# Attention and expert adapters on one core: how many whole-row stores may be on their way, row 5 and the end of row 7 stored in pieces, and a new order of the engines' work

## The chip, the cores and the metric

The kernel runs on one core of one Trainium2 chip. The metric is device time in microseconds (us) of one execution; less is better. The core's engines are PE (TensorE, matrix products; its weight loads are listed as PEld), ACT (ScalarE), DVE (VectorE), POOL (GpSimd) and SP (SyncE), and 16 DMA engines carry its transfers. Here POOL issues the loads of q, k and v, and SP issues the stores of the output.

## The reference, cut to what matters

```python
def _attn_ref(q, k, v):                      # (8, 8, 576, 64): batch, head, position, channel
    scores = np.matmul(q, k.transpose(0, 1, 3, 2)) / np.sqrt(D)
    # heads 0-3: rel = i - j in [0, 32); heads 4-7: rel in [0, 128) and rel % 4 == 0
    scores = np.where(mask, scores, -1e9)
    attn = softmax(scores)
    return np.matmul(attn, v)

def _moe_ref(x, w_gate, A, B):               # x: (8 * 576, 512), 8 experts of rank 16
    logits = x @ w_gate
    # the two largest logits of each token, softmax over these two -> w
    # out = x + sum over the two experts e of w_e * (x @ A[e]) @ B[e]
```

## The kernel before, in words

A *row* r (0 to 7) is one batch element: 576 tokens by 512 channels of float32, 1152 KB of output. A row has two halves g, the plain heads (g = 0) and the dilated heads (g = 1). All work is cut into named operations with an engine, a body and a list of operations that they wait for (`Program.add`, line 88). For a row r and half g:

- `L..`, `Lw..`, `Lq..`, `Lv..` load q, k and v from float32 in HBM to bfloat16 on the chip, issued by POOL. There are four input buffers, so row r uses that of row r - 4. Row 7 comes in eight pieces (lines 293 to 298): `Lq7gh` for queries and keys, `Lv7gh` for values. All of the pieces but `Lv700` and `Lv701` are put into the list `late`, and every store waits for that list.
- `S0`, `S1` (PE, scores), `E0`, `E1` (ACT, exponentials), `V` (PE, times the values), `R` and `N` (DVE, reciprocal and normalisation into the output tile X[r]), `B` (POOL, a bfloat16 copy of X[r]; the last part of row 7 is `Bx7` on ACT).
- `T`, `U` (PE, transposes), `C`, `Cd`, `Cp` (ACT, copies of them), `Z0`, `Z1` (PE, x times A and the gate), `Y0`, `Y1` (ACT, copies), then the gate's statistics on DVE: `m0`, `m1`, `s12`, `top`, `tt`, with `th` on ACT, `g2` on DVE; `gz` (POOL, gated z), `G` (PE, transposes), `gc` and `gn` (ACT, copies).
- `D0`, `D1`, `D2` (PE, times B): the first 1024 columns of half 0, those of half 1, and the last 128 columns of both halves. `A0`, `A1`, `A2` add them to X[r], on DVE; of rows 4 to 7 `A2` is done on POOL after a copy `dx` on ACT (lines 576 to 579). In the rows 5, 6 and 7 (`SHARED`, line 35) `A0` takes the first 512 columns only, and `A3` on POOL the next 512, after a copy `dy` on ACT (lines 554 to 559). In row 7 `D70` is for `A70` and `D73` for `A73`.
- `O` stores X[r], issued by SP, in the order O1 O0 O2 O3 O4 O5 O61 O60 O71 O70. Rows 0 to 5 go out whole (line 592) when `A0`, `A1`, `A2` (and `A3`) of the row are done. The rows 6 and 7 go out in halves of 576 KB (line 596); a half g waits for `Ag`, `A2` and, for g = 0, for `A3`.

The text PLAN (lines 602 to 633) gives the order of all operations. Each engine runs its own in that order, so an operation whose inputs are late holds up all behind it on its engine. The number after @ is the operation's first PSUM bank of eight; an operation that takes a bank waits for the users of the one that had it before (`ordered`, lines 96 to 114). Line 110 adds a wait to each store of a whole row:

```python
            if name[0] == "O":
                if len(name) == 2:
                    o.deps = o.deps + stores[-2:-1]
                stores.append(name)
```

So a whole-row store waits until the last store but one ahead of it has landed: O2 waits for O1, O3 for O0, O4 for O2, O5 for O3. SP issues in order, so a store that waits holds up those behind it.

Of the kernel before, what the change touches and what calls it, by code (L numbers as in the profile page):

```python
# [13 lines left out]
B, H, S, D = 8, 8, 576, 64  # L14
# [14 lines left out]
XG = 1152  # L29
# [52 lines left out]
class Program:  # L82
# [5 lines left out]
    def add(self, name, eng, work, emit, deps=(), bank=None):  # L88
        assert name not in self.ops, name
        o = Op(name, eng, work, emit, [d for d in deps if d is not None], bank)  # L90
        self.ops[name] = o
        if bank is not None:
            bank.users.append(name)
        return name

    def ordered(self, text):


        out, held, stores = [], [[] for _ in range(8)], []
        for word in text.split():  # L100
            name, _, at = word.partition("@")
            o = self.ops[name]
            if o.bank is not None and o.bank.users[0] == name:
                o.bank.at = int(at)
                for b in range(o.bank.at, o.bank.at + o.bank.size):
                    o.deps = o.deps + held[b]
                    held[b] = list(o.bank.users)
            if name[0] == "O":
                if len(name) == 2:
                    o.deps = o.deps + stores[-2:-1]  # L110
                stores.append(name)
            out.append(o)
        assert len(out) == len(self.ops) == len(set(o.name for o in out))
        return out
# [52 lines left out]
def program(nc=None, qkv=None, aw=None, bt=None, con=None, out=None):  # L167
    scale = 1.0 / float(D) ** 0.5
    pg = Program()
    add = pg.add  # L170

    def sb(name, shape, dt):
        return nc.alloc_sbuf_tensor(name, shape, dt) if nc is not None else None

    IN = [sb(f"in{i}", [128, SW], BF) for i in range(SLOTS)]
    X = [sb(f"x{r}", [128, 2 * XG], FP) for r in range(B)]
# [13 lines left out]
    G2 = [sb(f"g2{i}", [128, 5, 8], FP) for i in range(2)]  # L190
# [75 lines left out]
    qk_ready, v_ready, late = {}, {}, []  # L266
# [321 lines left out]
        adapters(r)  # L588
    for r in range(B):
        more = [f"A{r}3"] if r in SHARED else []  # L590
        if r < B - 2:
            add(f"O{r}", "SP", ("dma", 128, 9216), lambda r=r: [nc.sync.dma_start(out=out[r], in_=X[r][:, :])],
                [f"A{r}{n}" for n in range(3)] + more + late)
        else:
            for g in range(2):
                add(f"O{r}{g}", "SP", ("dma", 128, 4608), lambda r=r, g=g: [nc.sync.dma_start(
                    out=out[r][:, XG * g : XG * g + XG], in_=X[r][:, XG * g : XG * g + XG])],
                    [f"A{r}{g}", f"A{r}2"] + more * (1 - g) + late)
    return pg


PLAN = """
pz0 wz warm@4 F1@1 awf btf vz00 pz2 con vz10 Lk00 Lk01 Lv00 Lv01
S000@6 vz01 vz11 tab cc1 cd3 vz20 cc0 vz21 cd2 cd0 L11 pz1 E000
F2@1 L10 cd1 S100@4 S101@6 E100 E101 L2 Lw2 S001@2 E001 V00@4 R00 N00 V01@1
L3 Lw3 R01 F0@0 xz0 B00 N01 B01 T00@4 vz30 L4 Lw4 pz3 C00 S111@5 E111
awc S011@2 U0@0 T01@7 E011 V11@3 Cd0 Cp0 S010@1 C01 R11 vz31 E010 N11
Z00@0 Y00 m00 Z10@6 Y10 m10 S110@4 B11 s120 E110 tt0 th0 top0 V10@2
g20 gz0 T11@5 R10 N10 btc G0@1 gc0 D01@6 B10 gn0 D00@0 C11 xz1
U1@4 Cd1 Cp1 T10@5 C10 A01 A00 S121@6 E121 S120@3 S021@1 Z01@0 E021 Z11@5  # L610
Y01 m01 Y11 m11 L5 Lw5 s121 S020@1 D02@0 V21@5 E120 top1 tt1 th1 g21
E020 A02 V20@0 R21 N21 R20 gz1 G1@5 gn1 F3@6 S130@6 N20 gc1 B21 E130
S031@3 D12@2 E031 S030@0 D10@5 T21@7 E030 C21 A12 S131@3 B20 V30@0 A10 E131
U2@7 T20@6 R30 N30 Cp2 B30 L6 Lw6 V31@3 Cd2 C20 Z02@7 Y02 Z12@1 R31
N31 B31 T30@2 D11@6 Y12 C30 S041@4 A11 E041 S141@2 S140@6 m02 E141 S040@0
m12 s122 tt2 U3@5 Cp3 th2 E040 top2 Cd3 g22 gz2 V41@2 T31@0 E140
C31 V40@5 R41 N41 Z03@2 G2@0 Y03 gn2 Z13@1 gc2 R40 Y13 N40 B40
S051@2 D20@4 E051 A20 m13 S151@6 E151 Lq700 S050@0 S150@2 E150 m03 s123 V51@5
top3 tt3 T40@3 th3 Lq701 E050 C40 B41 g23 T41@4 C41 R51 Lq710 V50@0
N51 R50 D22@5 N50 U4@7 gz3 Cd4 Cp4 G3@6 gn3 D21@3 gc3 A22 A21  # L620
Z04@7 Y04 B50 Lq711 S060@0 D32@2 Z14@7 S161@5 m04 E060 Y14 m14 E161 s124
S160@0 A32 Lv710 T50@7 E160 D30@3 S061@5 top4 V60@0 A30 tt4 R60 C50 Lv711
O1 E061 B51 T51@3 N60 C51 V61@4 th4 g24 R61 N61 U5@7 S171@2 Cp5
Cd5 S070@0 Z05@7 E171 E070 Z15@6 Y05 S170@2 S071@4 Y15 Lv700 m05 m15 top5
Lv701 B60 gz4 E170 E071 s125 G4@0 B61 D31@6 tt5 th5 gn4 V70@1 T60@4
A31 gc4 V71@5 U6@0 C60 O0 g25 O2 gz5 G5@4 Cp6 Cd6 R70 N70
B70 T61@2 D41@0 D42@3 R71 N71 gn5 A41 C61 dx4 gc5 B71 Bx7 D40@5
Z06@2 Y06 Z16@4 Y16 A40 m06 A42 D52@3 m16 s126 dx5 top6 U7@7 Cp7
Cd7 tt6 T71@1 Cx7 C71 T70@4 D51@5 A52 th6 g26 A51 D50@0 A50 C70
gz6 Z07@2 Z17 m07 m17 s127 tt7 dy5 G6@5 gc6 O3 D61@0 th7 gn6  # L630
D62@7 A53 top7 O4 dx6 g27 D60@5 gy7 gz7 A62 dy6 O5 A61 A63
O61 G7@3 H7 gm7 gn7 gc7 D72@0 dx7 A72 D71@1 A60 D73@6 O60 A71
D70@7 O71 A70 dy7 A73 O70
"""

_INS = ["qkv", "aw", "bt", "con"]
# [64 lines left out]
```

## Time and profile before

| | us |
|---|---|
| median of 3 runs | 101.34 |
| lowest and highest | 100.81, 101.72 |
| profiled execution: span from the first to the last instruction | 99.2 |
| what lies around the span (101.34 - 99.2) | 2.1 |

| engine | busy us | share of the span |
|---|---|---|
| PE | 81.6 | 82% |
| ACT | 71.0 | 72% |
| DVE | 62.3 | 63% |
| POOL | 54.6 | 55% |

The profile tells no time of its own for the profiled execution beside its span. Its views count time from the span's start. A line of a group names the source line, the engine, the operation, output <- input and the number of instructions. In the page's slices one column is a fortieth of the span, 2.48 us; a busy digit is in tenths.

### The profile page before, as it was taken

The page shows a single profiled execution, that of the slowest core. Times are in us where ns is not written, and L with a number is a line of the kernel's source. Part 1 is how long each engine was busy: PE and PEld are TensorE (multiplying, and loading weights), DVE is VectorE, ACT ScalarE, POOL GpSimd, SP SyncE. Part 2 cuts the span into 40 slices and gives each one's busy share as a digit, 9 for nine tenths or more (in the row PEclk, how much of TensorE's full clock was granted, in tenths as well). Part 3 has the DMA queues.
Part 4 walks back from the last instruction along what each step waited for, and adds up shares of the span by engine and source line. Part 5 has one row for each costly group of instructions (what it writes and reads, how often), then busy time and mean ns, then how long its engine had stood idle before and what let it go on. Part 6 is the DMA issues. An engine that isn't in the chain of part 4 may idle for free.

```text
span 99.2 us, 3611 instructions
## 1 busy us (share of the span) xinstructions
PE 81.6 (82%) x1587; PEld 59.9 (60%) x1587; DVE 62.3 (63%) x138; ACT 71.0 (72%) x123; POOL 54.6 (55%) x73
## 2 busy tenths in 40 slices
PE   3999969959569989999897979999799989766200
PEld 2443457548356765779676859878687878545100
DVE  5770007706468189359746697779676999979700
ACT  5195494399938983896997679989689899757200
POOL 5999900880549136404942297099085574637800
PEclk9999999999999999999999999999999999999975
DMA  2999999999999999999999999999979988979991
GB/s 33 300 204 208 207 214 226 201 217 220 211 211 211 214 219 213 219 216 206 210 217 212 224 212 214 210 204 175 198 264 412 415 353 360 426 297 401 420 422 76
DMA packets 5807, 24.50 MB, mean 247 GB/s; under 512 B 800, under 2 KB 928, under 8 KB 5024
## 3 DMA queue, kind: packets, MB, share of 16 engines
q0 software_dynamic: 3920, 14.23, 71.9%
q1 hardware_dynamic: 1728, 9.77, 23.9%
q10 hardware_dynamic: 144, 0.28, 1.0%
q8 instruction: 12, 0.20, 0.7%
q14 instruction: 3, 0.02, 0.1%
HBM read 29.07 MB, written 9.44 MB: 388 GB/s over the span
## 4 chain that ended last, share of the span: by engine, by line
PE 57%; ACT 18%; DVE 9%; DMA 5%; issue 3%; POOL 2%; POOLq 0%
PE ps L213 49%; ACT p L351 11%; PE ps L414 5%; DMA out_dram<-x 5%; DVE x L551 4%; DVE x L390 3%; ACT xt L424 2%; PE ps L504 1%; ACT zs L472 1%; POOL x L559 1%; ACT in L263 1%; POOL xb L397 1%; PE ps L438 1%; ACT xt L427 1%; DVE top L492 1%
## 5 line engine op out<-in xcount | busy, mean ns | idle before, releaser
L397 POOL CAST xb<-x 128x1152 bf16<-128x1152 f32 (+1 forms) x16 | 18.3, 1144 | 25.4 <-DVE x L390 25.4
L351 ACT ACTIVATE p<-ps 128x960 bf16<-128x960 f32 (+1 forms) x32 | 27.6, 899 | 4.2 <-PE ps L213 4.1
L213 PE MATMUL ps<-in,p 128*64 128x130 bf16 (+1 forms) x416 | 21.5, 221 | 3.7 <-ACT p L351 3.1
L390 DVE TENSOR_TENSOR x<-ps,rec 128x1152 f32<-128x1152 f32 x16 | 21.7, 1358 | 0.5
L213 PEld LDWEIGHTS ps<-in,p 128*64 128x64 bf16 (+1 forms) x416 | 17.1, 104 | 7.2 <-ACT p L351 4.1
L551 DVE TENSOR_TENSOR x<-x,ps 128x1024 f32<-128x1024 f32 (+1 forms) x16 | 17.5, 1116 | 3.4 <-PE ps L213 3.4
L387 DVE RECIPROCAL rec<-ps 128x18 f32<-128x18 f32 x16 | 4.3, 270 | 17.5 <-PE ps L213 17.3
L213 PE MATMUL ps<-warm 128*128 128x512 f32 x22 | 13.1, 737 | 1.5 <-DVE warm L217 1.5
L499 POOL TENSOR_TENSOR gz<-zs,g 128x640 bf16<-128x640 f32 x7 | 8.9, 1275 | 9.4 <-DVE g L494 9.4
L213 PEld LDWEIGHTS ps<-in 64*64 64x64 bf16 x576 | 10.9, 106 | 2.9 <-issue 0.9
L213 PE MATMUL ps<-in 64*64 64x96 bf16 (+1 forms) x576 | 11.9, 201 | 0.7 <-issue 0.7
L273 POOL DMA_DIRECT2D in<-in_qkv_dram x22 | 11.8, 581 | 0.8 <-POOLq L684 0.8
L213 PE MATMUL ps<-aw,xt 128*128 128x136 bf16 x160 | 11.2, 223 | 0.1
L424 ACT COPY xt<-ps 128x1024 bf16<-128x1024 bf16 x8 | 8.1, 1011 | 3.4 <-PE ps L414 3.3
L213 PEld LDWEIGHTS ps<-aw,xt 128*128 128x128 bf16 x160 | 9.6, 98 | 0.9 <-ACT xt L424 0.4
L414 PE MATMUL ps<-one,xb 128*128 128x128 bf16 x128 | 9.6, 219 | 0.6 <-issue 0.5
L414 PEld LDWEIGHTS ps<-one,xb 128*128 128x128 bf16 x128 | 7.6, 97 | 2.0 <-POOL xb L397 0.7
L213 PEld LDWEIGHTS ps<-warm 128*128 128x128 f32 x22 | 4.8, 235 | 6.6 <-issue 5.0
L427 ACT COPY xt<-ps 128x1024 bf16<-128x1024 bf16 x7 | 7.2, 1033 | 1.5 <-PE ps L414 1.5
L213 PE MATMUL ps<-bt,gn 128*128 128x256 bf16 (+1 forms) x48 | 6.8, 263 | 1.6 <-ACT gn L523 0.8
L213 PE MATMUL ps<-bt,gc 128*128 128x256 bf16 (+1 forms) x48 | 6.6, 255 | 1.5 <-ACT gc L520 1.5
L472 ACT COPY zs<-ps 128x408 f32<-128x408 f32 (+1 forms) x14 | 5.9, 457 | 2.0 <-PE ps L213 2.0
(55 smaller groups left out, 101.8 us busy)
## 6 DMA issues: line engine op xcount, KB each, us to landing
out_dram<-x SPq DMA_DIRECT2D x6, 1152.0 KB, 6.1
in<-in_qkv_dram POOLq DMA_DIRECT2D x5, 1152.0 KB, 22.1
in<-in_qkv_dram POOLq DMA_DIRECT2D x10, 292.5 KB, 23.1
in<-in_qkv_dram POOLq DMA_DIRECT2D x10, 288.0 KB, 8.2
out_dram<-x SPq DMA_DIRECT2D x4, 576.0 KB, 3.8
in<-in_qkv_dram POOLq DMA_DIRECT2D x10, 146.2 KB, 8.1
in<-in_qkv_dram POOLq DMA_DIRECT2D x2, 434.2 KB, 13.7
awf<-in_aw_dram ACTq DMA_DIRECT2D x1, 272.0 KB, 3.8
```

Of the source, the lines that this page charges most:

```text
L213: return nc.tensor.matmul(o, lhsT=lhsT, rhs=rhs, start=start, stop=stop, skip_group_check=True)
L273: nc.gpsimd.dma_start(out=IN[r % SLOTS][half(a), at : at + n], in_=qkv[r, a, :, at - 2 * VB * a : at - 2 * VB * a + n],)
L351: return [nc.scalar.activation(p[:, :, :].rearrange("p h (s c) -> p h s c", c=PER)[:, :, b0 : b0 + nb, 0:SEG], PS[:, k.at : k.at + 2, 0 : ...
L387: rc = add(f"R{tag}", "DVE", ("el", 60), lambda: [nc.vector.reciprocal(rec[:, :].rearrange("p (b i) -> p b i", b=3), PS[:, k.at : k.at + 3 ...
L390: nm = add(f"N{tag}", "DVE", ("el", XG), lambda: [nc.vector.tensor_tensor(X[r][:, XG * g : XG * g + XG].rearrange("p (b i n) -> p b i n", ...
L397: add(f"B{tag}", "POOL", ("el", cut), lambda: [nc.gpsimd.tensor_copy(XB[r % 2][:, g, 0:cut], X[r][:, XG * g : XG * g + cut])], [nm] + free)
L414: nc.tensor.transpose(tp[j][:, 128 * u : 128 * u + 128], xb[:, g, 256 * u + 128 * j : 256 * u + 128 * j + 128], ident())
L424: return [nc.scalar.copy(xt[:, 0:2, 0:S].rearrange("p j (c i) -> p j c i", c=C)[:, :, :, 0:128], tp.rearrange("p j (i c) -> p j c i", c=C))]
L427: return [nc.scalar.copy(xt[:, 2:4, 0:512], tp)]
L472: zc.append(add(f"Y{st}{r}", "ACT", ("el", len(us) * ZW), lambda us=us, k=k: [nc.scalar.copy(zs[:, us[0] : us[-1] + 1].rearrange("p u n -> ...
L499: return [en.tensor_tensor(GZ[i][:, us[0] : us[0] + n, :].rearrange("p u (e r) -> p u e r", e=E), zv()[:, us[0] : us[0] + n, 0:ER].rearran ...
L551: return [nc.vector.tensor_tensor(v, v, PS[:, k.at : k.at + nk].rearrange("p b n -> p (b n)"), ALU.add)]
```

## The change

1. A whole-row store waits for the last store but two ahead of it: O3 waits for O1 and O4 for O0; O2 waits for no store.
2. Row 5 goes out in two halves, O51 (after `A51` and `A52`) ahead of O50 (after `A50`, `A52` and `A53`). Row 7's half 0 goes out in two pieces, O70 (its first 512 columns, after `A70` alone) and O70b (640 columns, after `A72` and `A73`). The order is O1 O0 O2 O3 O4 O51 O50 O61 O60 O70 O71 O70b.
3. PLAN is drawn up anew. The order of every engine is the same up to row 5's second scores (S150); up to there only banks differ. Behind it orders and banks differ.

```diff
@@ ordered
-                    o.deps = o.deps + stores[-2:-1]
+                    o.deps = o.deps + stores[-3:-2]
@@ program, stores
-        if r < B - 2:
+        if r < B - 3:
             add(f"O{r}", "SP", ("dma", 128, 9216), lambda r=r: [nc.sync.dma_start(out=out[r], in_=X[r][:, :])],
                 [f"A{r}{n}" for n in range(3)] + more + late)
         else:
             for g in range(2):
-                add(f"O{r}{g}", "SP", ("dma", 128, 4608), lambda r=r, g=g: [nc.sync.dma_start(
-                    out=out[r][:, XG * g : XG * g + XG], in_=X[r][:, XG * g : XG * g + XG])],
-                    [f"A{r}{g}", f"A{r}2"] + more * (1 - g) + late)
+                parts = ((0, XG, [f"A{r}{g}", f"A{r}2"] + more * (1 - g)),)
+                if (r, g) == (B - 1, 0):
+                    parts = ((0, 512, [f"A{r}0"]), (512, XG, [f"A{r}2"] + more))
+                for i, (x0, x1, made) in enumerate(parts):
+                    add(f"O{r}{g}" + "b" * i, "SP", ("dma", 128, 4 * (x1 - x0)), lambda r=r, x0=XG * g + x0, x1=XG * g + x1: [
+                        nc.sync.dma_start(out=out[r][:, x0:x1], in_=X[r][:, x0:x1])], made + late)
@@ PLAN, from row 5's second scores on
-S051@2 D20@4 E051 A20 m13 S151@6 E151 Lq700 S050@0 S150@2 E150 m03 s123 V51@5
-top3 tt3 T40@3 th3 Lq701 E050 C40 B41 g23 T41@4 C41 R51 Lq710 V50@0
-N51 R50 D22@5 N50 U4@7 gz3 Cd4 Cp4 G3@6 gn3 D21@3 gc3 A22 A21
-Z04@7 Y04 B50 Lq711 S060@0 D32@2 Z14@7 S161@5 m04 E060 Y14 m14 E161 s124
-S160@0 A32 Lv710 T50@7 E160 D30@3 S061@5 top4 V60@0 A30 tt4 R60 C50 Lv711
-O1 E061 B51 T51@3 N60 C51 V61@4 th4 g24 R61 N61 U5@7 S171@2 Cp5
-Cd5 S070@0 Z05@7 E171 E070 Z15@6 Y05 S170@2 S071@4 Y15 Lv700 m05 m15 top5
-Lv701 B60 gz4 E170 E071 s125 G4@0 B61 D31@6 tt5 th5 gn4 V70@1 T60@4
-A31 gc4 V71@5 U6@0 C60 O0 g25 O2 gz5 G5@4 Cp6 Cd6 R70 N70
-B70 T61@2 D41@0 D42@3 R71 N71 gn5 A41 C61 dx4 gc5 B71 Bx7 D40@5
-Z06@2 Y06 Z16@4 Y16 A40 m06 A42 D52@3 m16 s126 dx5 top6 U7@7 Cp7
-Cd7 tt6 T71@1 Cx7 C71 T70@4 D51@5 A52 th6 g26 A51 D50@0 A50 C70
-gz6 Z07@2 Z17 m07 m17 s127 tt7 dy5 G6@5 gc6 O3 D61@0 th7 gn6
-D62@7 A53 top7 O4 dx6 g27 D60@5 gy7 gz7 A62 dy6 O5 A61 A63
-O61 G7@3 H7 gm7 gn7 gc7 D72@0 dx7 A72 D71@1 A60 D73@6 O60 A71
-D70@7 O71 A70 dy7 A73 O70
+G2@4 Y03 gn2 Z13@2 gc2 R40 Y13 N40 B40 S051@0 D20@4 E051 A20 m13 S151@2
+E151 Lq700 S050@6 S150@0 B41 T41@2 E050 m03 s123 tt3 E150 th3 Lq710
+Lq711 top3 g23 V51@3 C41 U4@7 T40@6 gz3 R51 Cp4 V50@0 N51 Lq701 Cd4 B51
+Lv710 R50 N50 C40 G3@7 Lv711 Lv701 gn3 Z14@4 Y14 D21@5 A21 B50 O1 Lv700
+gc3 S060@3 E060 Z04@7 D22@0 A22 O0 O2 Y04 m04 m14 top4 S161@4 s124 tt4
+E161 S160@1 E160 th4 g24 gz4 S061@6 T51@3 D30@4 A30 E061 C51 V60@0 R60
+U5@6 Cp5 N60 Cd5 T50@7 C50 D32@3 V61@4 A32 R61 N61 S171@2 E171 S070@0
+E070 Z05@7 Y05 Z15@2 Y15 m05 m15 top5 s125 B60 tt5 S170@0 E170 D31@6
+S071@4 B61 A31 O3 th5 g25 V70@1 E071 G4@0 gn4 gz5 R70 N70 gc4 T60@4 C60
+V71@5 U6@2 Cp6 R71 Cd6 T61@1 C61 B70 N71 D42@0 G5@2 gc5 D41@3 A41 dx4
+A42 gn5 Z06@6 Y06 m06 Z16@7 Y16 T70@3 B71 m16 s126 Bx7 C70 top6 tt6 th6
+D40@0 A40 g26 gz6 T71@4 U7@2 Cd7 C71 Cx7 D51@6 A51 D50@0 Cp7 A50 O4
+D52@5 dx5 Z07@2 dy5 Z17 G6@5 gc6 D61@0 A52 O51 m07 m17 s127 tt7 th7 top7
+g27 gz7 gy7 gn6 D62@7 A61 D60@5 G7@3 A53 O50 H7 dx6 A62 O61 dy6 A63 gn7
+D70@0 gm7 gc7 D72@7 dx7 A60 O60 A70 O70 D71@4 A71 A72 O71 D73@3 dy7 A73
+O70b
```

## Rows read from the trace of the kernel before

**Rows 1.** The page: DMA busy in tenths and its rate in 40 slices; the instruction queue's transfers.

```profile
DMA  2999999999999999999999999999979988979991
GB/s 33 300 204 208 207 214 226 201 217 220 211 211 211 214 219 213 219 216 206 210 217 212 224 212 214 210 204 175 198 264 412 415 353 360 426 297 401 420 422 76
q8 instruction: 12, 0.20, 0.7%
```

**Rows 2.** Windows: length; PE, PEld, DVE, ACT, POOL busy us (count); clock, DMA share, GB/s.

```profile
73.00:86.00 13.00, 12.17 (x235) 9.84 (x227) 11.42 (x28) 12.45 (x26) 7.93 (x9) 1.00 0.95 394
76.00:81.00 5.00, 4.83 (x87) 3.92 (x84) 4.67 (x8) 4.63 (x10) 2.42 (x2) 1.00 1.04 433
81.40:82.40 1.00, 1.00 (x18) 0.96 (x17) 1.00 (x2) 1.00 (x3) 0.98 (x2) 1.00 0.40 166
87.80:88.90 1.10, 0.57 (x4) 0.31 (x4) 0.81 (x5) 1.10 (x3) 0.03 (x1) 1.00 0.44 184
97.00:97.50 0.50, 0.00 (x0) 0.00 (x0) 0.00 (x0) 0.00 (x0) 0.00 (x0) 0.50 0.42 166
97.50:98.00 0.50, 0.00 (x0) 0.00 (x0) 0.00 (x0) 0.00 (x0) 0.00 (x0) 0.50 0.07 28
```

**Rows 3.** One source line in windows, stores: all whole rows, O2, O4, O5, O70.

```profile
L592 SPq DMA_DIRECT2D out_dram<-x x6: 332/332/976, 72.4 to 87.9; - x6
DMA to landing us min/median/max: 4.4/6.1/8.6
...
L592 SPq DMA_DIRECT2D out_dram<-x x1: 332/332/332, 76.9 to 76.9; - x1
DMA to landing us min/median/max: 7.0/7.0/7.0
...
L592 SPq DMA_DIRECT2D out_dram<-x x1: 332/332/332, 83.9 to 83.9; - x1
DMA to landing us min/median/max: 6.3/6.3/6.3
...
L592 SPq DMA_DIRECT2D out_dram<-x x1: 333/333/333, 87.9 to 87.9; - x1
DMA to landing us min/median/max: 5.0/5.0/5.0
...
L596 SPq DMA_DIRECT2D out_dram<-x x1: 332/332/332, 94.3 to 94.3; - x1
DMA to landing us min/median/max: 4.1/4.1/4.1
```

**Rows 4.** What SP waited for from 77.3 to 84 us, and from 84.3 to 88 us: total, times, longest.

```profile
SPq L140 <- DMA out_dram<-x: 6.2, 2, 4.2
...
SPq L140 <- POOL x L559: 3.6, 1, 3.6
```

**Rows 5.** Timeline of DVE, then ACT, then POOL's A53, then SP's issue of O61.

```profile
76.37 1.22 DVE L551 TENSOR_TENSOR x<-x,ps 128x1024 f32<-128x1024 f32 x1 [0.20 <-PE ps L213]
...
80.94 2.34 DVE L551 TENSOR_TENSOR x<-x,ps 128x1024 f32<-128x1024 f32 x2
83.23 0.30 DVE L484 MAX8 mx<-zs 128x8 f32<-128x8 f32 x3
...
84.55 0.19 DVE L489 SCALAR_TENSOR_TENSOR tt<-zs,s 128x40 f32<-128x40 f32 x1
...
82.64 0.84 ACT L472 COPY zs<-ps 128x408 f32<-128x408 f32 x2
...
86.56 1.27 POOL L559 TENSOR_TENSOR x<-x,in 128x512 f32<-128x512 f32 x1
...
90.73 0.33 SPq L596 DMA_DIRECT2D out_dram<-x  x1
```

**Rows 6.** Timeline of POOL: B50, then three of row 7's loads.

```profile
64.49 1.14 POOL L397 CAST xb<-x 128x1152 bf16<-128x1152 f32 x1 [2.54 <-DVE x L390]
65.58 1.63 POOL L273 DMA_DIRECT2D in<-in_qkv_dram  x3
```

More of the change, by code:

```diff
@@ L599, in program @@
     return pg
 PLAN = """
[L603 to L616, printed above, removed]
@@ L617 @@
-C31 V40@5 R41 N41 Z03@2 G2@0 Y03 gn2 Z13@1 gc2 R40 Y13 N40 B40
-S051@2 D20@4 E051 A20 m13 S151@6 E151 Lq700 S050@0 S150@2 E150 m03 s123 V51@5
-top3 tt3 T40@3 th3 Lq701 E050 C40 B41 g23 T41@4 C41 R51 Lq710 V50@0
-N51 R50 D22@5 N50 U4@7 gz3 Cd4 Cp4 G3@6 gn3 D21@3 gc3 A22 A21
-Z04@7 Y04 B50 Lq711 S060@0 D32@2 Z14@7 S161@5 m04 E060 Y14 m14 E161 s124
-S160@0 A32 Lv710 T50@7 E160 D30@3 S061@5 top4 V60@0 A30 tt4 R60 C50 Lv711
-O1 E061 B51 T51@3 N60 C51 V61@4 th4 g24 R61 N61 U5@7 S171@2 Cp5
-Cd5 S070@0 Z05@7 E171 E070 Z15@6 Y05 S170@2 S071@4 Y15 Lv700 m05 m15 top5
@@ L633 @@
-D70@7 O71 A70 dy7 A73 O70
+pz0 wz warm@0 F1@3 awf btf vz00 pz2 con vz10 Lk00 Lk01 Lv00 Lv01 S000@4
+vz01 vz11 tab cc1 cd3 vz20 cc0 vz21 cd2 cd0 L11 pz1 E000 F2@7 L10 cd1
+S100@5 S101@0 E100 E101 L2 Lw2 S001@3 E001 V00@5 R00 N00 V01@1 L3 Lw3
+R01 F0@4 xz0 B00 N01 B01 T00@4 vz30 L4 Lw4 pz3 C00 S111@6 E111 awc
+S011@3 U0@2 T01@7 E011 V11@4 Cd0 Cp0 S010@1 C01 R11 vz31 E010 N11 Z00@3
+Y00 m00 Z10@0 Y10 m10 S110@1 B11 s120 E110 tt0 th0 top0 V10@2 g20 gz0
+T11@0 R10 N10 btc G0@5 gc0 D01@6 B10 gn0 D00@1 C11 xz1 U1@4 Cd1 Cp1
@@ new lines @@
+T10@0 C10 A01 A00 S121@6 E121 S120@3 S021@1 Z01@0 E021 Z11@7 Y01 m01 Y11
+m11 L5 Lw5 s121 S020@1 D02@0 V21@5 E120 top1 tt1 th1 g21 E020 A02 V20@0
+R21 N21 R20 gz1 G1@4 gn1 F3@5 S130@6 N20 gc1 B21 E130 S031@3 D12@2 E031
+S030@0 D10@5 T21@7 E030 C21 A12 S131@3 B20 V30@0 A10 E131 U2@7 T20@6 R30
+N30 Cp2 B30 L6 Lw6 V31@3 Cd2 C20 Z02@6 Y02 Z12@2 R31 N31 B31 T30@0 D11@6
+Y12 C30 S041@2 A11 E041 S141@4 S140@6 m02 E141 S040@0 m12 s122 tt2 U3@5
+Cp3 th2 E040 top2 Cd3 g22 gz2 V41@2 T31@0 E140 C31 V40@5 R41 N41 Z03@1
```

## The prediction

> **What bounds the kernel now.** I read the page's slices first. The 16 DMA engines are busy in nearly every slice [rows 1]: up to about 72 us with loads at some 210 GB/s, then with stores at 400 GB/s and more. The clock of PE stays at its full level until PE has nothing left to do [rows 2]. So the second view is of transfers: when each store is issued and when it lands [rows 3]. The first leaves at 72.4, when row 7's loads have landed, the last at 94.3, and it lands at 94.3 + 4.1 = 98.4; the span ends 0.8 later, at 99.2. Eight rows of 1152 KB (1.18 MB) at the undisturbed 433 GB/s of 76 to 81 us [rows 2] take 8 x 2.72 = 21.8 us. From the first issue to the last landing it was 26.0. What lies between is what a change of the stores can win.
>
> Third, the windows with little DMA [rows 2]. From 81.4 to 82.4 the share is 0.40, so 0.6 us is empty; from 87.8 to 88.9 it is 0.44, another 0.6. The view of SP's waits says why [rows 4]: O3 waited 4.2 us for O0, which lands 8.6 us after its issue, the longest of the six [rows 3]; O5 waited 3.6 us for POOL's A53, which ends at 86.56 + 1.27 = 87.8 [rows 5].
>
> Fourth, the end. In 97.0 to 97.5 the share is 0.42, in 97.5 to 98.0 it is 0.07, about one engine of 16 [rows 2]. So 15 engines have no data left at about 97.2 and one goes on. The landings tell that this one hardly waited before: O4 lands at 83.9 + 6.3 = 90.2, O5 at 87.9 + 5.0 = 92.9, O70 at 98.4: 2.7 us for one row, 5.5 for two, the pure transfer time. And O2 lands at 76.9 + 7.0 = 83.9 although most engines were empty from 81.5 on. A store lands with its slowest engine, and the slowest one is not idle in the gaps. Why it is behind can be bounded: 12 instruction transfers take 0.7% of 16 engines' 99.2 us [rows 1], so 11.1 / 12 = 0.93 us each, on one engine, while the other 15 go on.
>
> The Trainium skill ("Runtime: NRT & Kernel Launch", Instruction fetch mechanics) says that such blocks of 16 KiB come over a DMA queue of the sequencer's own, mostly hidden. The size agrees (0.20 MB in 12); hidden it would be for the engine that executes, and by it nothing would be added for a laggard, which takes 0.45 off the sum below.
>
> So two things share the bound: the DMA engines' work, and the times at which the compute engines hand over the rows 4 to 7.
>
> **A rule for the end.** O5 left at 87.9 with three rows to go. 3 x 2.72 = 8.2, and the 15 engines ended at about 97.2: the remaining 1.1 is 0.85 until the data moves (87.8 to 88.9 is empty for 0.62 after a last remnant) and small gaps of 0.25. So a store sets the end of the data at its issue + 0.85 + 2.72 for each row from it on. To that come 0.4 to land and a laggard, which before cost 98.4 - 97.2 - 0.4 = 0.8.
>
> **The change part by part.**
>
> *Loads.* Before, three of row 7's loads are issued at 65.58, behind the copy B50, which itself had waited 2.5 us for DVE [rows 6]. The slice of 67.0 to 69.4 shows 175 GB/s where 211 is usual [rows 1]: 36 x 2.48 = 89 KB, 0.4 us. In the new order B51 stands ahead of B50, and of the eight pieces only Lv700, for which no store waits, stands behind B50. At 0.54 us an issue (1.63 / 3) they pass in time; B50 comes up to 1.6 us later, and T50 behind it has been moved back behind T51. I take 0.4 us off the first store's issue (72.4 to 72.0), bounds 0 and 0.5. It counts at the end only if no gap opens later.
>
> *Three on their way.* O2 no longer waits for O1. Worth nothing: O1 and O0 still fill the engines from 73 on. O3 now waits for O1, which lands at 72.4 + 4.4 = 76.8, and for A31, done at 77.6 [rows 5]; its place in the order is about the same, so I keep it. SP is free for it, so the gap at 81.4 closes: 0.6 us for the 15 engines, between 0 and 0.6 for the last one. The data of O1, O0, O2, O3 then ends at about 72.0 + 0.85 + 4 x 2.72 = 83.7.
>
> *O4.* To go on without a gap it must leave at 83.7 - 0.85 = 82.9. Before it left at 83.9. It needs A40. Before, A41 and A40 run in one piece, 80.94 to 83.28, and row 6's statistics follow (m06 at 83.23, tt6 to 84.74) [rows 5]. In the new order A40 stands behind m06, m16, s126, top6 and tt6; these wait for ACT's Y06 and Y16, 82.64 to 83.48 before [rows 5]. If ACT stays where it was, the statistics end at 84.74, and A40, half of the pair's 2.34, at 85.9: upper bound 86.0. The lower one: ACT is busy 12.45 of 13 us from 73 to 86 [rows 2], so it can gain 0.55 and move Bx7 (0.6) behind Y06 and Y16: statistics at 83.6, A40 at 84.8. I take O4 at 85.2, nearer the lower, since Bx7 does stand behind both now. That opens a gap of 85.2 - 82.9 = 2.3 us on the 15 engines, in which a laggard catches up. End of the data: 85.2 + 0.85 + 4 x 2.72 = 96.9.
>
> *Row 5 in halves.* The bytes are the same, one issue of 0.33 us more on SP. Before, O5 waited for A53, at the end of POOL's chain A52, gz6, A53. Now O51 needs A51 and A52. POOL runs gz6, A52, A53: with A53 at 87.8 as before or up to 0.6 later, A52 is done at 86.6 to 87.2 (1.27 earlier). O51 at 87.2: 87.2 + 0.85 + 8.2 = 96.25. O50 at 88.4: 88.4 + 0.85 + 2.5 x 2.72 = 96.05. So the gap at 87.8 is gone as a bound.
>
> *Row 6.* O61 left at 90.73 [rows 5] behind Z07, Z17, row 7's statistics and A61, whose order is kept. It can come 0.6 earlier (ACT's idle time) or 1.0 later (row 5's late A40 stands ahead of Cx7 on DVE, and Z07 waits for Cx7). I take no shift: 90.7 + 0.85 + 2 x 2.72 = 97.0. This is the latest of all.
>
> *Row 7 in pieces.* O70 no longer waits for A72 and A73, one issue more. The last piece, 640 of 2304 columns, leaves when O70 did, 94.3: 94.3 + 0.85 + 0.28 x 2.72 = 95.9. Not a bound; it costs nothing unless POOL's A73 is 1.1 us late.
>
> *The rest of the order.* The work of PE, DVE, ACT and POOL is the same to the instruction; what it costs or gives is in the bounds of O4 and O61.
>
> **The sum.** Data ends at 97.0 by O61 (O4: 96.9) against 97.2. Landing 0.4. The laggard: between 0 (its instruction transfer falls into the gap ahead of O4) and 0.9 (behind it); I take 0.45. Last landing 97.85 against 98.4, so 0.55 less. By the profiled execution the span is 98.6 against 99.2; with the 2.1 around it, 100.8 against 101.34, which is the median, so the two go together. A measurement of this kernel tells about 1% (1.0 us) from no change.
>
> **The rivals.**
>
> *The engines never run dry (0.25).* A40 and Y06 come as early as ACT's idle time allows, O61 leaves at 89.7 to 90.1, and the empty 0.6 + 0.6 and the 0.4 of the loads all count: 101.34 - 1.6 = 99.8. For it: DMA is busy everywhere else. Against it: A40 has been put behind five operations.
>
> *The last engine decides (0.19).* Its transfers stood end to end before and its work is unchanged, so closing the others' gaps gives nothing: 101.3. For it: the landings' spacing of 2.7 a row. Against it: its lead of delay comes from single transfers of 0.93 us, which may hit another engine or a gap.
>
> *Row 4 comes too late (0.14).* The place is A40 behind the statistics of row 6. It decides from the point where O4's end passes the old one: t + 0.85 + 10.9 + 0.4 + 0.45 > 98.4, so t > 85.8; from there each us costs a us, since SP issues in order and all of the rows 5 to 7 follow. With ACT where it was and `top6` or D40 a us late, O4 leaves at 87.0: 102.5.
>
> *Each store pays a price of its own (0.01).* Two stores more, paid one after the other: before, O70's landing took 4.1 us for 1.36 us of data, 2.7 more, so 2 x 2.7 = 5.4: 106.7. Against it: the last four stores landed within 5.5 us of O5, the pure time of two rows' data. [...]
>
> **How the numbers follow.** My forecast, 100.8, has 0.41, its own range 100.2 to 101.6. Faster by over 1% (under 100.3): 0.24 of the first rival and 0.07 of my forecast's lower edge, 0.31. Slower (over 102.35): 0.09 of the third, 0.01 of the fourth and 0.03 of a tail that is late at O61, 0.13. Within 1%: 0.56. The range reaches to the first rival with 0.2 to spare and over most of the third: 99.6 to 102.2.
>
> **What would show it.** O3 issued at about 77, no low share at 81.4; a gap of 1 to 2.5 us ahead of O4's data between 83.7 and 86.5; O4 released by DVE's A40, not by a landing; the first store at 72.0; the last landing 0.4 to 1.3 us behind the moment when the DMA share falls. I am wrong if O4 leaves before 83.5 or after 86.5, if O61 moves by over 1 us, or if the landings of the last stores are spaced wider than 1.36 us a half.

## The result and the profile after

| | before | after |
|---|---|---|
| median of 4 runs, us | 101.08 | 104.65 |
| lowest and highest, us | 100.75, 101.72 | 103.83, 105.78 |
| profiled execution: span, us | 99.2 | 102.2 |

The change makes the kernel slower: the ratio is 1.0337, with an interval of 1.0286 to 1.0389. The forecast was 100.8 (99.6 to 102.2). The changed kernel was run a second time, beside other runs of the kernel before: 1.0444 [1.0337, 1.0550]. So about 3.6 us are to be found, and 3.0 of them are in the profiled execution. Ratios, here and below, are of executions in the faster of the two states that each kernel shows, so they can differ from the quotient of the medians; the profiled executions of the runs 5 and 9 fell in the slower state, and no reading of them is used.

The page of the kernel after, its DMA slices (a column is now 2.56 us), against [rows 1]:

```profile
DMA  2999999999999999999999999999599980699970
GB/s 40 307 211 205 206 211 230 215 202 216 206 220 214 212 221 207 219 207 215 221 212 211 216 216 210 213 208 182 218 418 404 436 368 36 288 399 420 414 318 13
q8 instruction: 12, 0.20, 0.7%
```

Up to the stores little differs. Then there is one deep hole (36 GB/s) where before there were two shallow ones, and at the end a slice of 13 GB/s. The windows of the kernel after, with the columns of [rows 2]:

```profile
82.00:84.00 2.00, 1.83 (x26) 1.42 (x25) 1.89 (x2) 2.00 (x5) 0.34 (x2) 1.00 1.04 433
84.00:86.00 2.00, 1.74 (x25) 1.32 (x23) 1.53 (x10) 2.00 (x5) 1.24 (x2) 1.00 0.15 60
86.00:88.00 2.00, 2.00 (x26) 1.39 (x25) 2.00 (x4) 1.67 (x6) 0.85 (x1) 1.00 0.17 74
88.00:90.00 2.00, 1.42 (x25) 1.25 (x22) 1.93 (x10) 1.32 (x4) 2.00 (x3) 1.00 1.04 433
...
98.50:99.00 0.50, 0.00 (x0) 0.00 (x0) 0.00 (x0) 0.00 (x0) 0.00 (x0) 0.50 1.05 420
99.00:99.50 0.50, 0.00 (x0) 0.00 (x0) 0.00 (x0) 0.00 (x0) 0.00 (x0) 0.50 0.20 74
99.50:101.40 1.90, 0.00 (x0) 0.00 (x0) 0.00 (x0) 0.00 (x0) 0.00 (x0) 0.50 0.05 20
```

The hole at 81.4 is closed, as forecast. The one ahead of row 4 lasts from 84.2 to 87.8. At the end 15 engines have no data left at about 99.1 (before 97.2), and then a share of 0.05, one engine of 16, goes on for 1.9 us more. By the landings of the last store on each of the 16 engines, the median goes from 97.61 to 99.45 and the last from 98.43 to 101.40. So of the 3.0 us, 1.84 are a later end of all, and 1.1 are a last engine that lags by 1.95 us where it lagged by 0.82.

The later end is in the hand-overs. SP's timeline of the kernel after, each line from a narrow window, in the order O3, O4, O61, O70b, against [rows 3, 5]:

```profile
79.13 0.33 SPq L592 DMA_DIRECT2D out_dram<-x  x1
...
86.98 0.33 SPq L592 DMA_DIRECT2D out_dram<-x  x1
...
92.55 0.33 SPq L601 DMA_DIRECT2D out_dram<-x  x1
...
96.35 0.33 SPq L601 DMA_DIRECT2D out_dram<-x  x1
```

O61 was at 90.73 and is at 92.55. By the prediction's own rule, 92.55 + 0.85 + 5.44 = 98.8, it sets the end of the data; O4 gives 86.98 + 0.85 + 10.88 = 98.7. Both are late. DVE's timeline shows what O4 waited for (row 6's statistics, then A40, the 128x1024 addition):

```profile
84.86 0.31 DVE L484 MAX8 mx<-zs 128x8 f32<-128x8 f32 x3 [0.44 <-ACT zs L472]
85.15 0.24 DVE L485 MAX8 mx<-zs 128x8 f32<-128x8 f32 x2
85.42 0.17 DVE L486 TENSOR_REDUCE s<-mx 128x5 f32<-128x10 f32 x1
85.50 0.19 DVE L492 TENSOR_TENSOR top<-zs,mx 128x40 f32<-128x40 f32 x1
85.62 0.20 DVE L489 SCALAR_TENSOR_TENSOR tt<-zs,s 128x40 f32<-128x40 f32 x1
85.74 1.21 DVE L551 TENSOR_TENSOR x<-x,ps 128x1024 f32<-128x1024 f32 x1
```

The order within is the one of the forecast; m06, the first line, came at 83.23 before and comes at 84.86. So what SP waits for is 1.6 to 1.8 us late from further up. PE's timeline shows where it starts: V60 (26 products), then U5 (2 products), with the idle time before it in brackets:

```profile
69.08 1.33 PE L213 MATMUL ps<-in,p 128*64 128x130 bf16 x26
72.09 0.27 PE L438 MATMUL ps<-one,xb 128*128 128x128 bf16 x2 [1.68 <-issue]
```

"issue" means that the profile shows nothing that PE waited for. The kernel before has such a line too, and the prediction overlooked it:

```profile
70.18 0.33 PE L213 MATMUL ps<-in,p 128*128 128x130 bf16 x3 [0.55 <-issue]
```

There PE stood 0.55 us inside V60, 1.9 us earlier. So PE's start is 1.9 us late, of which 1.1 us are a longer stand; PE also comes to the place 0.8 us later (72.09 - 1.68 = 70.41 against 70.18 - 0.55 = 69.63). The section on why the prediction was wrong takes the 0.8 apart.

### The profile page after: what moved, and what is told of

Read it like the earlier page. It is cut to its first block, busy times and chain, and to the rows that moved or that the text cites. A ratio compares the mean times of both kernels' runs of the same rounds, so it can differ in the third digit from the quotient of the medians.

```text
span 102.2 us, 3620 instructions
## 1 busy us (share of the span) xinstructions
PE 81.7 (80%) x1587; PEld 59.6 (58%) x1587; DVE 60.6 (59%) x138; ACT 71.4 (70%) x123; POOL 54.4 (53%) x73
## 3 DMA queue, kind: packets, MB, share of 16 engines
q0 software_dynamic: 3920, 14.23, 69.5%
## 4 chain that ended last, share of the span: by engine, by line
PE 46%; ACT 31%; DVE 7%; POOL 5%; issue 4%
PE ps L213 38%; ACT p L351 16%; PE ps L414 5%; POOL xb L397 3%; ACT xt L424 3%; ACT xt L427 3%; DVE x L390 3%; ACT zs L472 2%; ACT gn L523 2%; DVE x L551 2%; ACT gc L520 2%; POOL x L559 1%; PE ps L438 1%; ACT in L263 1%; PE ps L504 1%
## 5 line engine op out<-in xcount | busy, mean ns | idle before, releaser
(55 smaller groups left out, 99.6 us busy)
```

## The experiments

Two theories went into them. *The order*: its earlier loads, its late A40 or its banks cost the time. *The stores*: the rule for three on their way, or the smaller pieces, cost it.

**1. The stores alone.** The kernel before with the new rule, row 5 and row 7 in pieces, and only the names of the stores changed in PLAN (O5 becomes O51 and O50, O70b is added).

```diff
-                    o.deps = o.deps + stores[-2:-1]
+                    o.deps = o.deps + stores[-3:-2]
...
-        if r < B - 2:
+        if r < B - 3:
...
```

> The order of before, with the new rule of three stores on their way, O51 and O50, and O70 and O70b. Theory 1 (the new order makes rows 4 to 7 late, the stores are innocent): 100.2 to 101.2, no slower than before, because the gap at 81.4 closes and O51 leaves before A53. Theory 2 (three stores at once, or 12 instead of 10, cost transfer time of their own): 102 to 104.5.

Measured: 100.86 us against 100.81, a ratio of 1.0010 [0.9966, 1.0054]. O3 leaves at 77.51, O4 at 83.20, O51 at 86.29: earlier by 4.0, 0.7 and 1.6 us than O3, O4 and O5 before. But O61, which waits for no store, is at 90.61 (before 90.73), and the last landing is at 97.8 (before 98.4). The bytes that go out earlier only leave a new hole ahead of O61 (windows, columns of [rows 2]), and nothing is won that can be measured: the end hangs on O61.

```profile
88.00:90.00 2.00, 1.73 (x20) 1.25 (x21) 1.74 (x5) 1.44 (x5) 0.30 (x1) 1.00 0.97 399
90.00:91.50 1.50, 0.69 (x12) 0.43 (x9) 1.50 (x3) 1.08 (x4) 1.50 (x2) 1.00 0.23 92
```

**2. The order alone.** The new PLAN with the rule and the pieces of before.

```diff
-                    o.deps = o.deps + stores[-3:-2]
+                    o.deps = o.deps + stores[-2:-1]
...
-        if r < B - 3:
+        if r < B - 2:
...
```

> The new order with the old stores: two on their way, row 5 whole, row 7 in halves. Theory 1: 104.5 to 105.5, as slow as the changed kernel or a little slower. Theory 2: 101 to 102.5.

Measured: 103.55, a ratio of 1.0246 [1.0156, 1.0336]. That is less than the 104.5 to 105.5 expected if the order costs it, but well over the 101 to 102.5 of the other theory: the loss is the order's. PE stands 1.97 us at the same U5, and O61 leaves at 93.34.

**3. Row 7's loads late again.** The kernel after, in which POOL issues four of the loads behind B50, as the kernel before did with three.

```diff
-Lq711 top3 g23 V51@3 C41 U4@7 T40@6 gz3 R51 Cp4 V50@0 N51 Lq701 Cd4 B51
-Lv710 R50 N50 C40 G3@7 Lv711 Lv701 gn3 Z14@4 Y14 D21@5 A21 B50 O1 Lv700
+Lq711 top3 g23 V51@3 C41 U4@7 T40@6 gz3 R51 Cp4 V50@0 N51 Cd4 B51
+R50 N50 C40 G3@7 gn3 Z14@4 Y14 D21@5 A21 B50 Lq701 Lv710 Lv711 Lv701 O1 Lv700
```

> The changed kernel with Lq701, Lv710, Lv711, Lv701 issued behind B50, at about 66 us, so that the DMA engines run short for a moment as in the kernel before. Theory 1a (PE stands 1.7 us at 70.4 because its next 256 instructions come late over full DMA engines): the instruction transfer starts about 3 us after PE enters the previous block in place of 4.3, PE stands 0.6 us in place of 1.7, and the time falls by about 1 us to 103.5. Theory 1b (the wait for instructions has nothing to do with the loads, or rows 4 to 7 are late through their order alone): 104.3 to 105.

Measured: 102.45, a ratio of 1.0169 [1.0089, 1.0249], so about 2 us of the loss are gone, more than the 1 us expected. The order of PE is untouched, and U5 comes 2.0 us earlier. PE's and SP's timelines of this run (U5, O4, then the six stores from O51 to O71):

```profile
70.10 0.27 PE L438 MATMUL ps<-one,xb 128*128 128x128 bf16 x2 [0.57 <-ACT xt L427]
...
84.99 0.33 SPq L592 DMA_DIRECT2D out_dram<-x  x1
87.19 6.58 SPq L601 DMA_DIRECT2D out_dram<-x  x6
```

O4 at 84.99, O51 at 87.19, O50 at 88.41, O61 at 90.55: these are the forecast's 85.2, 87.2, 88.4 and 90.7. But the time is still 1.7% over. In the profiled execution the last engine lands at 99.41, 1.0 us later than before, when the median is at 97.46.

Not all of the 2.0 us is the edit's. The stand ahead of U5 is 1.1 us shorter (0.57 against 1.68); the other 0.9 PE had gained on the way there, 0.6 of it by 58.8 us, ahead of the first load that was moved (62.5 us in the kernel after). One such place is near 52 us, first in the kernel after, then in this run:

```profile
53.08 0.56 PE L414 MATMUL ps<-one,xb 128*128 128x128 bf16 x7 [1.09 <-issue]
...
51.95 0.56 PE L414 MATMUL ps<-one,xb 128*128 128x128 bf16 x7 [0.49 <-issue]
```

Up to there the two kernels are the same, so this difference is one between two executions.

The name in the bracket of U5 (an ACT copy) misleads. That copy ended at 70.02, but in run 6 below U5 starts at 70.67 although the same copy ends at 71.16, so U5 doesn't wait for it.

**4. The reverse.** The kernel before, with three of its loads issued ahead of B50.

```diff
-N51 R50 D22@5 N50 U4@7 gz3 Cd4 Cp4 G3@6 gn3 D21@3 gc3 A22 A21
-Z04@7 Y04 B50 Lq711 S060@0 D32@2 Z14@7 S161@5 m04 E060 Y14 m14 E161 s124
-S160@0 A32 Lv710 T50@7 E160 D30@3 S061@5 top4 V60@0 A30 tt4 R60 C50 Lv711
+N51 R50 D22@5 N50 U4@7 gz3 Lq711 Lv710 Lv711 Cd4 Cp4 G3@6 gn3 D21@3 gc3 A22 A21
+Z04@7 Y04 B50 S060@0 D32@2 Z14@7 S161@5 m04 E060 Y14 m14 E161 s124
+S160@0 A32 T50@7 E160 D30@3 S061@5 top4 V60@0 A30 tt4 R60 C50
```

> The kernel before with Lq711, Lv710, Lv711 issued at about 62 us, ahead of B50, so that the DMA engines never run short. Theory 1a: the first store leaves 0.4 us earlier, but PE stands over 1 us for instructions near 69.6 in place of 0.55; time up by 0.5 to 1 us, 101.6 to 102.1. Theory 1b: no longer wait, time 100.6 to 101.1.

The place at which PE stood 0.55 us before, now:

```profile
70.90 0.28 PE L213 MATMUL ps<-in,p 128*128 128x130 bf16 x2 [1.37 <-issue]
```

The stand grows by 0.8 us and O61 comes 0.7 later (91.45); the first store doesn't come earlier (72.44). The time doesn't move, 1.0001 [0.9959, 1.0044], while here the last engine hardly lags (98.41 against a median of 98.33, where before the lag was 0.82). So the longer stand and the later O61 are confirmed, but the time expected with them, 101.6 to 102.1, is not; the time alone would have spoken for the other theory.

**5 and 6. What the late loads leave.** Run 5 takes run 3 and does D40 and A40 ahead of row 6's statistics; run 6 takes run 3 and gives row 2's G2 the bank 3 in place of 4, for which D20 waited.

```diff
-A42 gn5 Z06@6 Y06 m06 Z16@7 Y16 T70@3 B71 m16 s126 Bx7 C70 top6 tt6 th6
-D40@0 A40 g26 gz6 T71@4 U7@2 Cd7 C71 Cx7 D51@6 A51 D50@0 Cp7 A50 O4
+A42 D40@6 A40 gn5 Z06@0 Y06 m06 Z16@1 Y16 T70@3 B71 m16 s126 Bx7 C70 top6 tt6 th6
+g26 gz6 T71@4 U7@2 Cd7 C71 Cx7 D51@6 A51 D50@0 Cp7 A50 O4
```

> The changed kernel with the loads behind B50 (after_loads_late, 102.45) and D40 and A40 ahead of row 6's statistics, in banks 6 and 7, with Z06 in bank 0 and Z16 in bank 1. O4 should leave at about 83.7 in place of 85.0. Theory 3 (row 4's late store sets what is left of the loss): down by about 1 us, 101.4. Theory 4 (15 engines are bound by O61 and the last one by an instruction transfer that comes behind the last gap): no gain, 102.2 to 102.9.

```diff
-G2@4 Y03 gn2 Z13@2 gc2 R40 Y13 N40 B40 S051@0 D20@4 E051 A20 m13 S151@2
+G2@3 Y03 gn2 Z13@2 gc2 R40 Y13 N40 B40 S051@0 D20@4 E051 A20 m13 S151@2
```

> after_loads_late with G2 in bank 3 in place of 4, so that D20 need not wait for ACT's copies of it (0.38 us on PE at 57). Theory 3 and 4: the tail of PE moves 0 to 0.4 us earlier, 102.0 to 102.5.

Measured: run 5 101.58, 1.0084 [1.0042, 1.0126], half of what was left, near the 101.4 of the theory that row 4's late store sets it (run 8 looks into that); run 6 103.02, 1.0215 [1.0142, 1.0288], over the 102.0 to 102.5 expected, so nothing is gained by the bank. In run 6 PE doesn't stand ahead of U5 at all, and yet U5 starts 0.57 us later than in run 3: near 52 us PE stood 1.09 us, as in the kernel after.

**7. Late loads with the old stores.** Run 3 with the rule and the pieces of before (the edit of run 2).

> after_loads_late with the old stores (two on their way, row 5 whole, row 7 in halves). Theory 4: row 5 as a whole leaves at about 88.4 and opens a gap in which the last engine catches up; its landing is 0.3 to 1 us behind the others in place of 1.9; 101.2 to 101.8. Theory 5 (the new order alone makes the last engine late): 102.3 to 103.

Measured: 102.49, 1.0216 [1.0122, 1.0311], against 102.45 in run 3. O61 leaves at 90.56 (run 3: 90.55). With the new order too the stores' part is worth nothing that can be measured. The gap ahead of the whole row 5 helped the last engine less than one theory expected (a lag of 0.3 to 1 us, 101.2 to 101.8): the lag is 1.25 us.

**8. Row 4 early alone.** The kernel after with the edit of run 5, its loads left early.

> The changed kernel with only D40 and A40 moved ahead as in late_row4_early; the loads as in the change, so PE should again stand 1.7 us for instructions at 70.4. O4 should leave at about 85.6 in place of 87.0. Theory 3: 103.4. Theory 1a and 4 (the whole tail is late, O61 at 92.5 binds as well): 104.0 to 104.7.

Measured: 103.07, 1.0145 [1.0044, 1.0245], less than either theory expected. The end of this run, in windows with the columns of [rows 2]:

```profile
98.50:99.00 0.50, 0.00 (x0) 0.00 (x0) 0.00 (x0) 0.00 (x0) 0.00 (x0) 0.50 1.03 409
99.00:99.50 0.50, 0.00 (x0) 0.00 (x0) 0.00 (x0) 0.00 (x0) 0.00 (x0) 0.50 0.63 246
99.50:101.40 1.90, 0.00 (x0) 0.00 (x0) 0.00 (x0) 0.00 (x0) 0.00 (x0) 0.50 0.00 0
```

This is the telling one. PE stands 1.68 us as in the kernel after, O61 is at 92.82 (0.3 later still), and the 15 engines end no earlier: 0.63 and 0.20 are the shares from 99.0 to 99.5. Yet the share of 0.05 behind them is gone, and with it about 1.5 us of the profiled execution (the last landing is at 99.84, not 101.40). The queues of a stretch show what differs. In the kernel after, from 91.0 to 92.6:

```profile
q1 hardware_dynamic: 156, 0.65, 99.5%
q8 instruction: 1, 0.02, 3.7%
```

In this run, from 89.0 to 90.3:

```profile
q8 instruction: 1, 0.02, 5.3%
q1 hardware_dynamic: 5, 0.01, 1.8%
```

The last instruction transfer (q8) falls among stores in the one (q1 at 99.5%), and into the hole ahead of O51 in the other (q1 at 1.8%), where few stores are on their way. The same for the other kernels, in order of the lag (the last landing less the median of the 16 engines), one profiled execution each:

| kernel | last instruction transfer, us | place | lag, us |
|---|---|---|---|
| 4, loads early before | 85.0 to 86.0 | ahead of the hole before O5 | 0.08 |
| 10, three edits | 84.6 to 85.5 | ahead of the hole before O51 | 0.10 |
| 8, row 4 early | 89.1 to 90.2 | in the hole before O51 | 0.15 |
| 1, stores alone | 84.2 to 85.9 | ahead of the hole before O61 | 0.34 |
| 12, other warm-up | 87.9 to 88.9 | in the hole before O4 | 0.36 |
| 2, order alone | 87.6 to 88.9 | end of the hole before O4, then one of 0.5 us | 0.61 |
| before | 85.0 to 85.9 | ahead of a hole of 0.6 us | 0.82 |
| 7, late, old stores | 89.3 to 90.2 | behind the last hole | 1.25 |
| 11, after again | 92.7 to 93.7 | behind the last hole | 1.88 |
| 6, late, bank 3 | 90.3 to 91.2 | behind the last hole | 1.95 |
| 3, late | 89.3 to 90.3 | behind the last hole | 1.95 |
| after | 91.3 to 92.2 | behind the last hole | 1.95 |

**9 and 10. Towards a better version.** Run 9 is run 1 with `Lq710` also behind B50, to thin the loads further. Run 10 is the kernel after with the edits of 3, 5 and 6 together.

```diff
-top3 tt3 T40@3 th3 Lq701 E050 C40 B41 g23 T41@4 C41 R51 Lq710 V50@0
+top3 tt3 T40@3 th3 Lq701 E050 C40 B41 g23 T41@4 C41 R51 V50@0
...
-Z04@7 Y04 B50 Lq711 S060@0 D32@2 Z14@7 S161@5 m04 E060 Y14 m14 E161 s124
+Z04@7 Y04 B50 Lq710 Lq711 S060@0 D32@2 Z14@7 S161@5 m04 E060 Y14 m14 E161 s124
```

> The order of before with the new stores (stores_alone, 100.86), and Lq710 too behind B50, so that four loads are issued from 65.3 on and the DMA engines run short from about 65.6 to 66.9. Theory 1a: the instruction transfer for PE's block at 69 starts at about 66.5 in place of 67.7, PE does not stand there (0.82 in stores_alone), the rows 5 to 7 come 0.5 us earlier, and the loads end 0.5 us later, which O61 hides: 100.2 to 100.6, faster than before. Theory 1b: no change of the wait, the later loads cost 0 to 0.5: 100.9 to 101.4.

> The changed kernel with all three repairs: loads behind B50, D40 and A40 early, G2 in bank 3. If the wait for instructions and the last engine are all that makes the new order slower, it is as fast as before: 100.5 to 101.3. If the order loses something else, over 101.5.

Measured: run 9 1.0019 [0.9979, 1.0059], no gain, where 100.2 to 100.6 was expected. Run 10 101.06 against 100.71, 1.0051 [1.0016, 1.0086]: nearly all of the loss is undone, and its last engine isn't late. No version beat the kernel before.

**11. The changed kernel again**, without an edit.

> The changed kernel once more, for a second profile. If the wait for instructions belongs to this order of loads it comes again: PE stands 1.4 to 2 us near 70 us, O4 leaves at 86.5 to 87.5, the last landing is 1.5 to 2 us behind the others. If it was chance, PE stands 0.5 us and the time is near 102.5. Time 103.8 to 105.

Measured: 105.49, the ratio of 1.0444 given above. Its profiled execution has both losses once more: PE stands 2.24 us ahead of U5, and the last engine lands at 102.81, with a median of 100.93. But O4 leaves at 88.46 and the time is over the 103.8 to 105 expected, for a third loss comes in, which the profiled execution of the kernel after doesn't have: PE's granted clock falls to its lower level (1.2 GHz) at 73.8, behind the stand, and is back at 2.4 GHz at 77.2 (windows, columns of [rows 2]; the clock is the third number from the end).

```profile
60.00:73.70 13.70, 11.03 (x253) 9.02 (x249) 9.17 (x20) 10.37 (x20) 8.59 (x11) 1.00 0.97 202
73.80:77.20 3.40, 3.40 (x62) 2.73 (x61) 1.63 (x2) 1.73 (x3) 0.60 (x1) 0.50 1.01 417
```

From PE's start behind the stand to O61 it is 21.8 us here (72.18 to 94.03) and 20.6 in the kernel after (71.99 to 92.55), so the fall goes with about 1.3 us.

**12. Does PE wait for its instructions?** The kernel after with another warm-up: one wide product at the start gives way to eight narrow ones. Every later product is then 28 instructions further back in PE's stream, and nothing else changes.

```diff
-            mm(bank(k), w, w[:, 0:1].to_broadcast([128, 512]), True, True) for _ in range(n)][:0], after, k)
+            mm(bank(k)[:, 0:c], w, w[:, 0:1].to_broadcast([128, c]), True, True)
+            for c in ([512] * n if n != 5 else [512] * 4 + [64] * 8)][:0], after, k)
```

> The changed kernel with only the warm-up altered: of its five wide products at the start four stay, and eight narrow ones (64 columns) take the place of the fifth, so every later product of PE stands 28 instructions of PE further back in its stream (each of these float32 products shows as two products and two weight loads), and the tail's order is untouched. Theory 'PE waits for its own instructions at a fixed count': the stand of 1.65 us ahead of U5 goes to an earlier place of the order, 28 instructions before, which is in the middle of V60 (12 of its 26 products done, 14 to come), where no other engine hands anything over; it is 1.0 to 2.3 us long there, nothing or under 0.3 us is left ahead of U5, O61 leaves at 91.5 to 93.2 and the time stays within 1.2 us of the changed kernel's. Rival 'U5 waits for something of its own that the profile does not show': the stand stays ahead of U5 and V60 runs through in 1.3 us as before.

PE's timeline of this run, V60 in two parts and U5 (now at line 439), and PE's waits without a named cause from 60 to 99 us (total, times, longest):

```profile
69.48 0.59 PE L213 MATMUL ps<-in,p 128*64 128x130 bf16 x12
71.54 0.93 PE L213 MATMUL ps<-in,p 128*64 128x130 bf16 x14 [1.46 <-issue]
72.31 0.27 PE L439 MATMUL ps<-one,xb 128*128 128x128 bf16 x2
```

```profile
PE ps L213 <- issue: 2.7, 3, 1.5
```

V60 is cut after exactly 12 of its 26 products, and U5 follows without a wait. So PE stands at a count of its own instructions, not at something that U5 needs. Counted along PE's recorded instructions from 0, the one that starts behind this place is number 2497 in all 11 kernels of the table in which PE stands there: a product of V60 before, the start of U5 in the kernel after, the weight load of V60's 13th product here. The time of the one execution, 103.81, is as expected, but O61 missed its range: 93.91, not 91.5 to 93.2. The other two waits of the last line are 0.39 us at 65.5 and 0.80 us at 84.1, ahead of the instructions 2241 and 3009, that is 256 before and 512 behind. That the time is no worse fits the lag of 0.36 us in the table.

The trace's records of the instruction queue give the rest. In the 12 kernels of the table PE's first instruction behind this place starts 1.24 to 1.58 us after the end of the transfer before it: 70.64 and 71.99 in the kernel after, 68.93 and 70.18 before, 68.59 and 69.99 in run 3, 70.79 and 72.18 in run 11. The transfer's end itself lies anywhere from 68.5 to 71.5. So PE's start follows the transfer (run 6 alone says nothing of it, since PE doesn't stand there), and the transfer was 1.7 us later than before. The queues of 66.0 to 69.5 us in run 3, with more of its loads behind B50, have the transfer in them:

```profile
q0 software_dynamic: 206, 0.64, 101.2%
q8 instruction: 1, 0.02, 1.7%
```

The same stretch of the kernel after has none, and more of the loads (q0); its transfer starts at 69.7:

```profile
q0 software_dynamic: 249, 0.73, 105.5%
```

## Why the prediction was wrong

**The step that failed first is O61, "no shift", bounds -0.6 and +1.0, and with it the sentence that the rest of the order is "in the bounds of O4 and O61".** O61 moved by 1.8 us. The working counted each engine's work and its inputs, and found both unchanged. It had no term for PE waiting for its own instructions, although the 0.55 us of "issue" stood in the trace before. The new order moved row 7's loads ahead of B50, which the prediction put down as a gain of 0.4 us. The first store did come a little earlier (72.17 against 72.36), but the next instruction transfer came 1.7 us later, and PE, ACT and DVE with it. Runs 3 and 4 show the load order making this stand shorter and longer, run 12 that it is at a count of instructions.

From PE's start behind the stand to O61 it takes the same 20.6 us in both kernels (70.18 to 90.73, 71.99 to 92.55), so the whole shift of 1.8 is made ahead of that. Up to 58.8 us PE is level (instruction 1985 starts at 58.74 before and at 58.80 in the kernel after). From there 0.38 is lost up to instruction 2241 (64.99 and 65.43), 0.24 of it one more stand, at that count, which run 11 of the same kernel doesn't have; 0.35 by the new order itself, whose stretch from there to the stand takes 4.99 us where the old one takes 4.64, and does so in run 3 with late loads as well (64.54 to 69.53); the rest, 1.0 to 1.1, is the longer stand. So 1.3 of the 1.8 us are waits for instructions, and 0.35 is what the prediction had put at nothing under the rest of the order.

**O4 left its bounds.** Forecast 85.2 (84.8 to 86.0), measured 86.98; the prediction itself had named a time over 86.5 as proof that it was wrong. The term's own mechanism was right: A40 stands behind row 6's statistics, and with the loads put back it leaves at 84.99 (85.96 in run 6). What was wrong is that the bounds were taken from ACT's idle time alone, as if nothing further up could move. The rival "row 4 comes too late" had O4 at 87.0 and 102.5 us; O4 came there, by another cause, and its price left out the other losses.

**The laggard was mis-sized.** The mechanism stood in the prediction: between 0, if its instruction transfer falls into the gap ahead of O4, and 0.9, if behind it. The table fits that, but behind the last hole it costs 1.25 to 1.95 us. The 0.9 was the length of the transfer itself. In the kernel after the lag is 0.8 us at O4 and 2.1 at O51: 1.3 more, where the transfer itself takes 0.94. It may be more still, for the transfer starts at 91.30 and O4's last landing, 91.82, is behind that: in run 12, whose transfer lies in the hole ahead of O4, the lag at O4 is 0.15.

**What held.** The hole at 81.4 closed and paid nothing; the 433 GB/s; the rule issue + 0.85 + 2.72 a row (98.8 by O61, 99.1 in the windows); the last piece of row 7 (96.35 + 0.85 + 0.76 = 98.0) isn't a bound. In run 3 the hand-overs came within 0.2 us of the forecast, with some luck: in run 6, with the same loads, O4 and O61 are at 85.96 and 91.52, still in their bounds. The 0.4 us for the earlier loads came out as 0.19, and the slice of low rate that it was read from is there in the kernel after too (182 GB/s from 69.0 to 71.6). That two more stores pay no price of their own is shown by run 1 and by runs 3 and 7. Apart from that and the new order's 0.35, the forecast was a sum of right terms for a kernel whose instructions come as before.

The sum of the loss in the profiled execution: O61 later by 1.82, the lag larger by 1.13, together 2.9 of the 3.0 us.

**What stays open.** What sets the moment of an instruction transfer is not known. No run moves the last one alone, so that its place makes the lag is read from the table, not shown by an edit. Ahead of U5 it starts 2.4 to 4.8 us after PE enters the stretch of 256 instructions before, with early loads 3.5 to 4.8 and with late ones 2.4 to 3.6; that fuller load queues hold it up is argued from runs 3 and 4, not shown by itself. The last transfer of the kernel after comes 6.3 us later than before, and why is open too. So is what made PE's clock fall in run 11: in run 2 it stayed at 2.4 GHz behind a stand of 1.97 us. In run 10 the stand is still 1.15 us with late loads, so the order of the loads isn't all of it. The 0.5% by which run 10 is over the kernel before has no cause shown.

## What to carry to other kernels

Before moving loads or stores in a kernel whose DMA engines are full, look for idle time of the busiest engine that the profile gives to "issue" and for the instruction queue's few transfers: such an engine may be waiting for its own instructions, and an order that is better for the data can make these later. A hand-written order should be judged with its loads moved separately, in both directions. Where stores end a kernel, take the landing of the last engine apart from that of the others, since one small transfer behind the last gap can show up in full at the end.

## What the hardware showed unexpectedly

- PE stood 0.30 to 2.24 us in 11 of the 12 kernels, with its data there, at a fixed count of its instructions, and went on 1.24 to 1.58 us after a 16 KB transfer of the instruction queue had ended. The Trainium skill ("Runtime: NRT & Kernel Launch", Instruction fetch mechanics) calls the cost of such a crossing mostly hidden. These traces disagree where the DMA engines are full: in the kernel after, 1.68 us of it are in plain sight.
- Where such a transfer of 0.94 us fell among the last stores, the lag of the last DMA engine grew by 1.3 us or more, and the kernel's stores ended with that engine, 1.95 us after the median.
- Behind a stand of 2.24 us PE's granted clock fell to 1.2 GHz for 3.4 us (run 11), which went with 1.3 us of the time; in the other kernels of the table it stayed at 2.4 GHz behind the stands.
- Closing holes of the DMA engines was worth nothing: run 1 has only one of 0.3 us between 73 and 90 us, and its ratio is 1.0010 [0.9966, 1.0054].
